# Score passes of two heads together, a ring of 30 tiles, late checks by threes, and the router inside the stream of tiles

## The reference, cut to what matters

```python
# q, k, v: (2, 8, 576, 64) float32; w_gate: (512, 8); w1: (8, 512, 1024); w2: (8, 1024, 512)
scores = q @ k.transpose(0, 1, 3, 2) / 8
kth = np.partition(scores, -32, axis=-1)[..., -32:-31]        # the 32nd largest of a row
scores = np.where(scores >= kth, scores, -1e9)
attn = np.exp(scores - scores.max(-1, keepdims=True))
attn = attn / (attn.sum(-1, keepdims=True) + 1e-9)
x = (attn @ v).transpose(0, 2, 1, 3).reshape(1152, 512)

logits = x @ w_gate
expert = argmax(logits, axis=1)                               # the first of equals
gate = softmax(logits)[expert]                                # of the chosen expert
# tokens go to their experts in order; an expert takes at most 288, the rest are dropped (zero rows)
y = maximum(x_of_expert @ w1[e], 0) @ w2[e]
out[token] = gate * y
```

## Time and profile before

| | us |
|---|---|
| three runs | 514.79, 522.92, 529.53 (median 522.92) |
| the profiled execution, its own time | 516.76 |
| its span | 515.0 |
| busy: PE / weight loads / DVE / ACT / POOL | 441.0 / 374.4 / 286.5 / 244.4 / 251.2 |
| tiles, until the last normalisation begins | 310.3 |
| routing, scatter and load of rows, until the first transposes of experts | 338.1 |
| experts, until the end | 515.0 |

### The profile page before, as it was taken

How to read it: one execution, slowest core, us unless ns; L and a number is a source line. 1 busy time by engine, 2 the same in 40 slices (tenths; PEclk the granted TensorE clock), 3 DMA queues, 4 the chain that set the end, 5 groups by cost and what they waited for, 6 DMA issues and landing times.

```text
span 515.0 us, 8992 instructions
## 1 busy us (share of the span) xinstructions
PE 441.0 (86%) x2901; PEld 374.4 (73%) x2901; DVE 286.5 (56%) x1401; ACT 244.4 (47%) x419; POOL 251.2 (49%) x269
## 2 busy tenths in 40 slices
PE   3992379999899998999989993069999999999992
PEld 2561157777677776777878882069999999999992
DVE  1799999999989989899923204000212121222222
ACT  2361378867788687889758750012121131222220
POOL 3244599987799687999865550300011020220122
PEclk9996579979999799999989896559999999999998
DMA  4121010120286601000010020399995666878300
GB/s 102 37 60 33 1 37 11 23 48 2 57 244 162 200 34 24 3 14 12 1 25 1 1 94 0 124 330 330 333 336 193 211 224 215 300 254 279 109 19 12
DMA packets 53893, 57.89 MB, mean 112 GB/s; under 512 B 33102, under 2 KB 35150, under 8 KB 53840
## 3 DMA queue, kind: packets, MB, share of 16 engines
q1 hardware_dynamic: 51568, 52.50, 33.0%
q0 software_dynamic: 2272, 4.73, 2.7%
HBM read 45.39 MB, written 14.18 MB: 116 GB/s over the span
## 4 chain that ended last, share of the span: by engine, by line
PE 42%; DVE 4%; DMA 2%; POOL 2%; issue 2%; ACT 0%; SPq 0%; DVEq 0%; POOLq 0%
PE ps_s L635 15%; PE ps_s L650 14%; PE ps_o L527 5%; PE ps_t L498 2%; PE ps_o L615 2%; PE ps_t L605 2%; PE ps_s L538 1%; DMA dispatched<-x,r_slot 1%; PE ps_s L554 1%; DMA scores<-dispatched 1%; DVE next L847 1%; DVE below L866 1%; DVE cand L812 1%; POOL rest L382 1%; POOL out_dram L439 0%
## 5 line engine op out<-in xcount | busy, mean ns | idle before, releaser
L527 PE MATMUL ps_o<-v_aug,pT 128*128 128x128 f32 (+5 forms) x800 | 121.4, 292 | 0.0
L387 POOL TENSOR_TENSOR probs<-scores,probs 128x576 f32<-128x576 f32 x72 | 101.0, 1410 | 34.5 <-ACT probs L712 29.3
L527 PEld LDWEIGHTS ps_o<-v_aug,pT 128*128 128x128 f32 (+3 forms) x800 | 102.6, 187 | 13.8 <-issue 6.8
L382 POOL TENSOR_TENSOR rest<-below,scores 128x576 f32<-128x576 f32 x72 | 100.0, 1407 | 17.1 <-DVE below L866 17.1
L439 POOL DMA_INDIRECT out_dram<-yo,numbers x24 | 22.0, 915 | 161.0 <-DVE yo L1046 160.4
L481 PE MATMUL ps_s<-kT,qT 64*128 64x288 f32 x256 | 81.9, 455 | 16.2 <-ACT scores L687 15.4
L635 PE MATMUL ps_s<-scores,w_sb 128*128 128x192 f32 (+4 forms) x512 | 79.6, 311 | 0.6 <-ACT scores L765 0.6
L812 DVE MAX8 cand<-scores 128x8 f32<-128x96 f32 x432 | 72.1, 243 | 13.5 <-ACT scores L687 13.5
L635 PEld LDWEIGHTS ps_s<-scores,w_sb 128*128 128x128 f32 x512 | 75.7, 196 | 0.9 <-ACT scores L765 0.9
L650 PE MATMUL ps_s<-scores,w_sb 128*128 128x192 f32 (+4 forms) x512 | 74.5, 304 | 0.0
L650 PEld LDWEIGHTS ps_s<-scores,w_sb 128*128 128x128 f32 x512 | 71.9, 190 | 0.0
(11 more groups left out here) (102 smaller groups left out, 319.8 us busy)
## 6 DMA issues: line engine op xcount, KB each, us to landing
w_sb<-in_moe_w_dram SPq DMA_DIRECT2D x15, 2048.0 KB, 10.2
dispatched<-empty SPq DMA_DIRECT2D x18, 257.0 KB, 6.1
scores<-dispatched SPq DMA_DIRECT2D x24, 192.8 KB, 3.6
out_dram<-empty SPq DMA_DIRECT2D x9, 256.0 KB, 3.1
q_nat<-in_q_dram SPq DMA_DIRECT2D x16, 128.0 KB, 2.3
k_nat<-in_k_dram SPq DMA_DIRECT2D x16, 128.0 KB, 2.4
v_aug<-in_v_dram SPq DMA_DIRECT2D x16, 128.0 KB, 2.4
w_sb<-in_moe_w_dram SPq DMA_DIRECT2D x4, 512.0 KB, 7.8
```

What stands on the lines that cost most here:

```text
L382: nc.gpsimd.tensor_tensor(rest[:, n % 3, :], below[:, n % 3, :], score_tile(n), ALU.mult).then_inc(rest_ready, 1)
L387: nc.gpsimd.tensor_tensor(probs[:, n % PROBS, :], score_tile(n), probs[:, n % PROBS, :], ALU.subtract).then_inc(masked_ready, 1)
L527: last = nc.tensor.matmul(dst, lhs, v_aug[0:keys, g % 2, c, h, 0:width], start=(c == 0), stop=(c == TT - 1))
```

## The change

- The scores of pair 0 are made as before. From pair 1 on, tile r of both heads is made in one pass (`qk_heads`), at steps with s % 9 in 0, 2, 4, 6; the tail tile comes last (`qk_tail`). The order of making within a pair is then 0, 5, 1, 6, 2, 7, 3, 8, 4 (`made_at`, `tile_made`), while VectorE, GpSimd and the later stages keep the order of tiles. A pass waits until both banks are copied.
- LEAD is 22, the ring holds 30 tiles. The next pair's q and k are transposed at s % 9 == 6. The masks of GpSimd keep their groups up to group 20 and then come by four: behind the last pick come the masks from 59 on.
- Pairs 0 to 5 are checked as before; pairs 6 and 7 in threes, so there are 12 checks. The first four checks of these six lie in groups 20 to 23, the fifth behind `search_rest(23)`, the last behind `normalise(6, 0)`.
- Chunks 0 to 6 of x are transposed, copied and multiplied in the stream, behind the weighted values of tiles 18, 27, 36, 45, 58, 66 and 68 (TURNED), through `ps_t` and a buffer `xT`; the logits go to spare columns of the bank of the weighted values, and VectorE adds them up in `normalise` (`add_logits`).
- In the queue of SyncE several flags' gathers go ahead of loads of v, as the diff shows, and q and k of pair 7 go ahead of the fill of `dispatched`, which goes ahead of the flags of pair 4 as before.
- The buffer of w1 lies in the ring of scores.

```diff
-    LEAD = 18
-    HELD = 21
-    ROUTED = [0, 2, 4, 6, 10, 12, 16]
+    LEAD = 22
+    HELD = 30
+    NEXT = 6
+    CHOSEN = 20
+    PAIRWISE = PAIRS - 2
+    CHECKS = PAIRWISE + 3 * (PAIRS - PAIRWISE)
+    ENDING = 3 * PAIRWISE
+    TURNED = {TILES * 2: 0, TILES * 3: 1, TILES * 4: 2, TILES * 5: 3, TILES * 6 + FULL: 4,
+              TILES * 7 + FULL - 1: 5, TILES * 7 + FULL + 1: 6}
+    SPARE = FULL * (D + 1) + P
...
+        w1_sb = carve(2 * CH * F).rearrange("p (u c f) -> p u c f", u=2, c=CH)
...
+        def made_at(n):
+            g, t = divmod(n, TILES)
+            if g == 0:
+                return t
+            return TILES * g + (2 * t if t < FULL else 2 * (t - FULL) - 1 if t > FULL else TILES - 1)
...
             gather_bad(1)
-            load_v(2)
             load_qk(5)
             gather_bad(2)
-            load_v(3)
+            load_v(2)
             load_qk(6)
             gather_bad(3)
+            load_v(3)
+            load_qk(7)
             sp.wait_ge(empty_ready, 4)
             for n in range(E * CAP // P):
                 sp.dma_start(disp[n * P:(n + 1) * P, :], empty[:, :]).then_inc(drams_filled, 16)
+            gather_bad(4)
             load_v(4)
-            load_qk(7)
-            gather_bad(4)
             for n in range(N // P):
                 sp.dma_start(out[n * P:(n + 1) * P, :], empty[:, 0:DM]).then_inc(drams_filled, 16)
+            gather_bad(5)
             load_v(5)
-            gather_bad(5)
-            load_v(6)
             gather_bad(6)
             gather_bad(7)
+            load_v(6)
+            for i in range(8, CHECKS - 1):
+                gather_bad(i)
             load_v(7)
+            gather_bad(CHECKS - 1)
...
+                due = 3 * (m - 3) if m <= ENDING + 2 else 3 * (m - 3) + m - ENDING - 2
+                if masked < due:
+                    mask(masked)
                 if m < GROUPS - 1:
                     push_down(3 * m + 2)
+                for n in range(masked + 1, due):
+                    mask(n)
+                masked = max(masked, due)
+            for n in range(masked, ALL):
+                mask(n)
...
+            def qk_heads(g, r):
+                if r == 0:
+                    pe.wait_ge(nat_copied, 2 * (g + 1))
+                pe.wait_ge(s_ready, TILES * g + 2 * r)
+                for half in range(2):
+                    keys = slice(half * HALF, (half + 1) * HALF)
+                    for h in range(2):
+                        last = nc.tensor.matmul(ps_s[:, h, half, 0:HALF], qT[h * D:(h + 1) * D, g % 2, r * P:(r + 1) * P],
+                                                kT[h * D:(h + 1) * D, g % 2, keys], start=True, stop=True)
+                        if half == 1:
+                            last.then_inc(s_in_psum, 1)
...
+            def transpose_x(n, transposed):
+                b, c = divmod(n, CH)
+                pe.wait_ge(x_ready, 2 * (n + 1))
+                pe.wait_ge(pT_copied, transposed)
+                if n > 0:
+                    pe.wait_ge(xr_copied, n)
                 for t in range(TT):
                     rows = P if t < FULL else TAIL
-                    last = nc.tensor.transpose(XR[:, t * P:t * P + rows],
+                    last = nc.tensor.transpose(ps_t[:, t * P:t * P + rows],
...
+                done = s - LEAD - 4
+                if done in TURNED:
+                    transpose_x(TURNED[done], min(ALL, done + 2))
+                if done - 1 in TURNED:
+                    logits(TURNED[done - 1])
...
+                    for i in range(CHECKS):
+                        if m == (3 * i + 4 if i < PAIRWISE else i - PAIRWISE + ENDING + 2):
+                            if j == 1:
+                                counted = count_bad(i)
+                            if j == 2:
+                                recheck(i, counted)
...
+            def add_logits(n):
+                dve.wait_ge(logits_done, n + 1)
+                total = r_log[:, n // CH]
+                if n % CH == 0:
+                    nc.vector.tensor_copy(total, LOG[n]).then_inc(log_read, 1)
+                else:
+                    dve.wait_ge(log_read, n)
+                    nc.vector.tensor_tensor(total, total, LOG[n], ALU.add).then_inc(log_read, 1)
...
+                if m == GROUPS:
+                    normalise(PAIRS - 3, 1)
                 if m > 0:
                     search_rest(m - 1)
+                if m == GROUPS:
+                    recheck(CHECKS - 2, count_bad(CHECKS - 2))
...
-            normalise(PAIRS - 3, 1)
-            recheck(PAIRS - 1, count_bad(PAIRS - 1))
+            normalise(PAIRS - 2, 0)
+            recheck(CHECKS - 1, count_bad(CHECKS - 1))
             dve.wait_ge(consts_ready, 11)
-            normalise(PAIRS - 2, 0)
             choose_experts(0)
```

More of the change, by code:

```diff
@@ L468, in load_and_transpose, with qk_first @@
                 transpose_nat(k_nat)
-            def qk(n):
-                g, t = divmod(n, TILES)
-                if t == 0:
-                    pe.wait_ge(nat_copied, 2 * (g + 1))
-                if n >= 2:
-                    pe.wait_ge(s_ready, n - 1)
+            def qk_first(t):
+                if t >= 2:
+                    pe.wait_ge(s_ready, t - 1)
                 for half in range(2):
                     keys = slice(half * HALF, (half + 1) * HALF)
-                    dst = ps_s[:, n % 2, half, 0:HALF]
-                    if t != FULL:
-                        h, r = (0, t) if t < FULL else (1, t - FULL - 1)
-                        last = nc.tensor.matmul(dst, qT[h * D:(h + 1) * D, g % 2, r * P:(r + 1) * P],
-                                                kT[h * D:(h + 1) * D, g % 2, keys], start=True, stop=True)
-                    else:
-                        for h in range(2):
-                            last = nc.tensor.matmul(dst[h * TAIL:(h + 1) * TAIL, :],
-                                                    qT[h * D:(h + 1) * D, g % 2, FULL * P:S],
-                                                    kT[h * D:(h + 1) * D, g % 2, keys], start=True, stop=True)
@@ new lines, in qk_first @@
+                    for h in heads_of(t):
+                        r = FULL if t == FULL else t - h * (FULL + 1)
+                        dst = ps_s[h * TAIL:(h + 1) * TAIL, t % 2, half, 0:HALF] if t == FULL else ps_s[:, t % 2, half, 0:HALF]
+                        last = nc.tensor.matmul(dst, qT[h * D:(h + 1) * D, 0, r * P:min(S, (r + 1) * P)],
+                                                kT[h * D:(h + 1) * D, 0, keys], start=True, stop=True)
+                last.then_inc(s_in_psum, 1)
[7 more added lines that the diff above has]
+                        last = nc.tensor.matmul(ps_s[:, h, half, 0:HALF], qT[h * D:(h + 1) * D, g % 2, r * P:(r + 1) * P],
+                                                kT[h * D:(h + 1) * D, g % 2, keys], start=True, stop=True)
+                        if half == 1:
+                            last.then_inc(s_in_psum, 1)
@@ new lines, in qk_tail @@
+            def qk_tail(g):
+                pe.wait_ge(s_ready, TILES * g + TILES - 2)
+                for half in range(2):
+                    keys = slice(half * HALF, (half + 1) * HALF)
+                    for h in range(2):
+                        last = nc.tensor.matmul(ps_s[h * TAIL:(h + 1) * TAIL, 0, half, 0:HALF],
+                                                qT[h * D:(h + 1) * D, g % 2, FULL * P:S],
+                                                kT[h * D:(h + 1) * D, g % 2, keys], start=True, stop=True)
@@ L491, in transpose_probs @@
                 pe.wait_ge(exp_ready, n + 1)
+                turned = sum(1 for at_tile in TURNED if at_tile <= n - 2)
+                if turned > 0:
+                    pe.wait_ge(xr_copied, turned)
                 pe.wait_ge(nat_copied, 2 * naturals)
@@ L528, in weighted_values @@
                 last.then_inc(pv_done, 1)
+            def transpose_x(n, transposed):
[4 more added lines that the diff above has]
+                    pe.wait_ge(xr_copied, n)
+                for t in range(TT):
+                    rows = P if t < FULL else TAIL
+                    last = nc.tensor.transpose(ps_t[:, t * P:t * P + rows],
+                                               x[0:rows, t, b * PITCH + c * P:b * PITCH + (c + 1) * P],
+                                               ident[0:rows, 0:rows])
+                last.then_inc(xr_in_psum, 1)
             def logits(n):
```

166 lines of the change are left out of this document (86 added, 80 removed).

## The result

The changed kernel takes 521.52 us (median of 20 runs, 517.42 to 525.13), the kernel before 516.04 us in as many runs on the same chips (510.94 to 529.53): a ratio of 1.0157 with a 95% interval of 1.0125 to 1.019. It is slower by more than its measurement is uncertain. I had forecast 518.0 and, on one profiled execution, a gain of 0.9 us: the time lies in my range, and it moved the other way. The profiled executions differ by 5.7 us of span, 520.7 against 515.0.

What follows compares the result with a forecast made beforehand. TensorE and VectorE were taken to share the bound while tiles flow. Terms +2.3 to the last pick, -3.8 in the drain and +0.6 gave -0.9 us, 515.9 profiled; forecast 518 with two added for the median, range 503 to 530.

Steps and rivals of the forecast that it cites:

- Flag 4 then goes behind it in queue and data ... I take 4 us: SyncE's queue: flag 4 lands late behind the fill of dispatched, so VectorE waits 4 us, bounds 0 and 6.1.
- Four loads go behind flags, harmlessly: SyncE's queue: four loads issued behind flags' gathers instead of ahead of them cost nothing.
- The natural transposes come two steps later ... at no cost: TensorE's stream: transposes of the next pair's q and k move two steps later, costing nothing.
- Gains and costs of TensorE cancel in the middle: Middle pairs: paired passes save 3.4 us, router chunk and bubble add 2.0 and 0.7; TensorE 30.1 against VectorE 30.2.
- rival of no overlap: Paired passes don't overlap: TensorE takes 33.5 us a pair of heads; 519, or 525 with clock falls; chance 0.11.
- Check 5 at 202.5 + 0.6 + 4 + 1: VectorE's check 5: undisturbed time plus two logits, flag and clock gives 208.1, 1.6 us earlier than before.
- The 7.2 us that VectorE lost behind the lag: Checks 1 to 5 before: VectorE loses about ScalarE's lag behind the checks less 5 us, 7.2 us in all.
- Clock: Middle pairs: TensorE's granted clock falls in all four instead of two, 3.2 us each; slower, 524.0; chance 0.14.
- Lead 22, ring of 30 ... this gives 0: Middle: gates move four steps later, only copies of scores run further ahead, VectorE waits nowhere for scores: 0 us.
- Checks by threes: Pairs 6 and 7: six checks for two, 1.1 us each in the stream; three more before the last pick, 3.3 us.
- the drain: Last pick to last normalisation: two steps less -4.0, one router chunk less -2.0, bubbles +2.2; together -3.8 us.
- TensorE starts it rested, as now: Stretch after the last pick: TensorE begins at the lower clock as before, so the clock's 3.1 us stay.

Runs made afterwards that it cites:

- the test with flag 0 in front: Changed kernel with flag 0's gather issued ahead of the loads of q and k for pair 3: 516.9 us, ratio 1.0047.
- The half-width test: Changed kernel with the fill of dispatched in two halves of columns, one issued earlier, one left ahead of flag 4: 512.84 us in one run.
- the version with both edits: Changed kernel with the fill ahead of v 3 and q and k 7, and flag 0 ahead of q and k 3: 509.81 us, ratio 0.9907.
- single passes: Changed kernel with both queue moves, but single-head score passes in the old tile order instead of pairs: 521.42 us, ratio 1.0154.
- Short chunks: Changed kernel with both queue moves; router chunks 0 to 3 take only the first of five row tiles: only checks read, check 5 at 203.59.
- the kernel before with its load moved: Kernel before, with only the loads of q and k for pair 7 moved ahead of the fill of dispatched: 530.73 us, ratio 1.033.

## Why the prediction was wrong, by its own steps

**"Flag 4 then goes behind it in queue and data ... I take 4 us": the failed step, in size.** The mechanism was the one forecast, and even its place. The size is 9.26 us, above my upper bound of 6.1. Two numbers were off. The transposes at step 51 let the load of q and k go at 158.9, where I had put 154, so the fill was issued until 176.4 and not 171. And for the flag's landing I took 6 us behind the last issue, the median over all 18 parts; it was 9.4. VectorE wanted the flag at 176.6 and not at 173 to 174, which gave some 3 us back. The median of the parts says little of what stands behind the last of them: they land 3.5 to 9.0 us after their issues. Issues and timeline of the changed kernel:

```profile
dispatched<-empty SPq DMA_DIRECT2D x18, 257.0 KB, 6.2
```

```profile
164.89 11.47 SPq L314 DMA_DIRECT2D dispatched<-empty  x18
176.41 1.68 SPq L291 DMA_DIRECT2D bad_row<-bad  x1
```

Windows of the changed kernel (last columns: DMA share, GB/s):

```profile
165.00:170.00 5.00, 4.95 (x38) 3.56 (x37) 4.93 (x39) 3.07 (x6) 4.96 (x4) 1.00 0.87 267
170.00:175.00 5.00, 5.00 (x42) 4.44 (x40) 4.96 (x17) 5.00 (x9) 4.02 (x6) 1.00 1.07 281
175.00:180.00 5.00, 4.92 (x39) 4.01 (x38) 1.55 (x10) 4.09 (x7) 5.00 (x5) 1.00 1.07 269
180.00:185.00 5.00, 5.00 (x38) 3.69 (x36) 0.00 (x0) 0.82 (x2) 1.32 (x1) 1.00 1.15 264
```

An estimate by bytes over rate comes nearer: 18 parts of 257 KB are 4.7 MB, which at the 270 GB/s of these windows take 17.5 us from 164.9, until 182.4, not 11.5. The flag landed at 185.8, 3.4 us later. In the test with flag 0 in front the same estimate, at its 311 GB/s, gives 179.0, and the flag landed at 182.4, again 3.4 later. The kernel before moved 288 and 283 GB/s in the windows of its fill from 150 to 160, so its trace already had a rate for it. The half-width test bears out that it is the bytes: the same number of DMAs, half the bytes, 0.46 us. What the 3.4 us are, beside the 1.9 that a flag takes with nothing ahead of it, no run separates; v of pair 4 is issued in this time.

**"Four loads go behind flags, harmlessly": wrong for what it left out.** I had looked at loads that moved, and not at one that stayed ahead of flag 0 in both kernels: q and k of pair 3, which wait for the transposes of pair 2. **"The natural transposes come two steps later ... at no cost"** fails with it. In the kernel before pair 2's run at 33.7 and the loads are over long before the flag; in the changed one they run at 47.3, two steps later and behind a slow start of the paired passes (last section). The flags were found at 51.9 and the DMA issued at 55.4. I had this at nothing; check 0 came 3.1 us later than in the kernel before (54.38), and 3.4 later than with flag 0 in front (54.13), where the late transposes cost nothing.

**"Gains and costs of TensorE cancel in the middle": right.** The passes save what I had said: eight instructions in 1.24 us, against 1.2.

```profile
218.88 1.24 PE L521 MATMUL ps_s<-kT,qT 64*128 64x288 f32 x8
```

By the page on tiling that the prediction names (the Trainium skill, TensorEngine Tiling (Array Packing), Tiling Modes), tiles of 64 rows and 128 columns are independent; this trace agrees. The router's chunk came at the size forecast (transposes 0.83 us, logits 1.27). What a pair of heads takes from gate to gate where no check holds ScalarE is seen in the version with both edits, whose gates come some 5 us behind their checks (timeline of ScalarE):

```profile
180.15 0.22 ACT L761 ACTIVATE edge<-thr 128x9 f32<-128x9 f32 x1
...
210.48 0.22 ACT L761 ACTIVATE edge<-thr 128x9 f32<-128x9 f32 x1
```

That is 30.3 us with a chunk of the router in it, and 28.2 without one (88.47 to 116.64), against my 30.1. VectorE's period there is 30.0. So the two are level, as I had them, although TensorE is busy for only 112.7 of the 120 us from 86 to 206: with single passes, where it does hold the others up, it is busy for 113.3 of the same 120. Short chunks change nothing because VectorE is as long; single passes take 3.4 us a pair back and cost 12 to 14 us. My rival of no overlap, 519 to 525 us for a profiled execution, has what that test gives (523.71); it came without a late flag.

**"Check 5 at 202.5 + 0.6 + 4 + 1".** Without the late flags it is 205.26 and 203.50 in two profiles, against 204.1 without my 4 us. The 7.2 us that VectorE lost behind the lag went, as said. Gates follow their checks by 3.0, 1.9, 2.7, 1.5 and 1.9 us in the changed kernel, inside the forecast 1 to 5. **Clock:** in the changed kernel its column drops in three of the four pairs from check 1 to check 5 (to 0.78 from 130 us, 0.71 from 160, 0.66 from 190), where it had dropped in two. That is as often as my rival asked for, but not at its price. With a drop, the version with both edits takes 31.8 us from gate to gate (116.64 to 148.42) in place of 30.3, 1.5 us more and not the 3.2 of the kernel before, where the column went to 0.50; and VectorE's periods in the changed kernel stay at 29.9 and 30.3 beside the flag's wait.

**"Lead 22, ring of 30 ... this gives 0": wrong in its reason.** "Only copies of scores run further ahead" hides that the new order of tiles needs the lead. With 18 the kernel takes 28.8 us of span more than with 22. The 0 held only for lead and order taken together.

**"Checks by threes" and the drain.** From check 5 to the last pick's mask I forecast +3.9; measured +3.0 (6.4 to 9.4). The drain from there: -3.8 forecast, -4.1 measured (44.2 against 48.3 us). The last step, from there to the end: +0.6 forecast, +0.5. "TensorE starts it rested, as now", so at the lower clock, holds in the changed kernel: the granted clock is 0.50 from 274 to 278 us, and the weighted values of tile 59 take 4.39 us for 20 instructions, against 2.82 at full clock. This is the 1.9 us that mask 59 ahead of the last pick saves.

In sum: -0.9 forecast, +5.7 measured. Flag 4 waits 5.3 us longer than I had it and flag 0 brings VectorE 3.1 late, so -0.9 + 5.3 + 3.1 = +7.5; the other 1.8 went to the good side, 0.4 up to check 5, 1.0 up to the last pick and 0.4 behind it. The split between the flags is one of counting: both meet at check 4, which comes when flag 4 lands, however early VectorE is.

## What to carry to other kernels

A tiny DMA on which an engine waits must be placed by what stands ahead of it in its queue: each wait of an earlier load, and all bytes of an earlier fill over the measured rate, not the median landing of one part. Two such DMAs, late behind something in their queue, cost 12 us here and turned a change that is 0.9% faster into one that is 1.6% slower. When a load is moved, list every small transfer that it passes, and see when the load's own wait ends in the new order of work; do the same for loads that stay where they are. And a part that comes out at nothing (the lead) can still carry another (the order): only a test without it shows that.

## What the runs showed of the hardware that I had not expected

**A DMA of 0.5 KB behind 4.7 MB took 9.4 us to land**, 6.6 in the test with flag 0 in front and 4.0 in the kernel before with its load moved, where four loads of v stood between; it took 1.9 to 2.3 us where the fill was over. SyncE's issues take longer too with more bytes: 18 of them 11.47 us at 257 KB each and 8.99 at half of that. Why, no run shows. The flag's own issue of 1.68 us (0.52 elsewhere) is no sign of it: behind the same fill it took 0.58 in the test with flag 0 in front.

**Matmuls at half speed under a granted clock of 1.00.** At the start of the changed kernel (timeline of TensorE):

```profile
41.48 2.29 PE L521 MATMUL ps_s<-kT,qT 64*128 64x288 f32 x8 [1.27 <-ACT scores L746]
...
45.04 2.29 PE L521 MATMUL ps_s<-kT,qT 64*128 64x288 f32 x8 [1.27 <-ACT scores L746]
47.27 1.41 PE L484 MATMUL ps_t<-ident,q_nat 128*128 128x128 f32 x5
```

The same eight instructions take 1.24 us later on, the transposes 0.86. The kernel before takes the same 1.41 us for such transposes where the clock's column reads 0.50 (timeline of TensorE and window of the kernel before):

```profile
69.34 1.41 PE L454 MATMUL ps_t<-ident,q_nat 128*128 128x128 f32 x5
...
65.00:70.00 5.00, 4.03 (x16) 2.30 (x17) 5.00 (x29) 4.11 (x7) 4.70 (x7) 0.50 0.00 0
```

In the changed kernel the column reads full speed (window of the changed kernel):

```profile
35.00:45.00 10.00, 6.25 (x24) 3.09 (x20) 9.87 (x55) 3.57 (x6) 5.65 (x7) 1.00 0.02 4
```

A paired pass waits until both score banks are copied, and ScalarE for the pass: 3.56 us for two tiles, where the kernel before had 1.02 for one. The longer pass is 1.05 us of that, and the copies between passes 1.27. Such durations last up to some 76 us, so the mean clock of a span (0.938 here) counts this stretch as full speed. Why the column and the durations part, no run shows; the durations are what the path pays.
